# Pooled attention and two feed-forward layers on one core: the opening redone, attention stages reordered, a pass's weights fetched before it

## What is computed

```
attention (B=8, H=8, S=576, D=64):  k_p, v_p = mean of k, v over groups of 8 rows        (72 rows left)
    p = softmax(q k_p^T / sqrt(D));  attended = p v_p        -> x, 4608 tokens x 512
layer 1:  h = x w_in;   y = (h * sigmoid(h)) w_out            (512 -> 2048 -> 512)
layer 2:  h = y w_in2;  out = (h * clip(h + 3, 0, 6) / 6) w_out2
```

## Time and profile before

| | |
|---|---|
| median of 3 runs | 1788.66 us (1784.32 to 1789.85) |
| profiled execution, its own time | 1785.52 us |
| its span, first to last instruction | 1783.4 us |
| busy: PE, DVE, ACT, POOL | 96%, 58%, 41%, 17% |
| mean granted clock of PE | 0.977 |

### The profile page before, as it was taken

The page is one execution under the profiler, slowest core; times in us unless marked ns, Lnnn a source line. Parts: engine busy times, 40 slices in busy tenths (PEclk is TensorE's granted clock), DMA queues, the critical chain, the costliest instruction groups (busy, mean ns, idle before and its releaser), DMA issues. The chain is left out here.

```text
span 1783.4 us, 27222 instructions
## 1 busy us (share of the span) xinstructions
PE 1703.2 (96%) x10992; PEld 1518.4 (85%) x10992; DVE 1041.1 (58%) x1578; ACT 728.3 (41%) x1180; POOL 307.3 (17%) x421
## 2 busy tenths in 40 slices
PE   5778999999999999999999999999999999999999
PEld 4668788788788989999999889999999899999998
DVE  6745565565465456555555765555555776666664
ACT  3544454454454443333333444433444533333332
POOL 3563254254220240000000320000001400000000
PEclk7889999999999999999999999999999999999999
DMA  7232243243221232222222231111112332212221
GB/s 172 75 106 82 82 112 89 81 118 97 81 84 45 95 119 71 72 83 81 86 95 90 75 107 48 48 48 48 48 48 71 92 122 71 71 71 71 77 78 60
DMA packets 130293, 145.95 MB, mean 82 GB/s; under 512 B 47992, under 2 KB 74872, under 8 KB 130168
## 3 DMA queue, kind: packets, MB, share of 16 engines
q1 hardware_dynamic: 80424, 128.08, 22.2%
q10 hardware_dynamic: 49744, 16.13, 3.6%
HBM read 96.99 MB, written 47.19 MB: 81 GB/s over the span
## 5 line engine op out<-in xcount | busy, mean ns | idle before, releaser
L992 DVE TENSOR_TENSOR x_sum<-xy,x_sum 128x256 f32<-128x256 f32 x144 | 60.7, 422 | 227.7 <-ACT x_sum L749 227.7
L1025 DVE TENSOR_TENSOR g_lo<-g_raw,g_hi 128x1024 fp32r<-128x1024 f32 x144 | 184.2, 1281 | 6.4 <-ACT g_raw L761 6.4
L531 PE MATMUL xy<-xr_hi,w1r_hi 128*128 128x256 f32 x576 | 167.8, 291 | 11.7 <-DVE x_sum L992 6.3
L749 ACT COPY x_sum<-xy 128x256 f32<-128x256 f32 x144 | 52.5, 366 | 299.7 <-PE xy L533 299.6
L605 PE MATMUL acc<-g_hi,w_hi 128*128 128x512 f32 x400 | 173.3, 433 | 0.0
L532 PE MATMUL xy<-xr_lo,w1r_hi 128*128 128x256 f32 x576 | 163.6, 284 | 0.0
L533 PE MATMUL xy<-xr_hi,w1r_lo 128*128 128x256 f32 x576 | 163.6, 284 | 0.0
L606 PE MATMUL acc<-g_lo,w_hi 128*128 128x512 f32 x400 | 162.1, 405 | 0.0
L607 PE MATMUL acc<-g_hi,w_lo 128*128 128x512 f32 x400 | 161.3, 403 | 0.0
L1016 DVE TENSOR_TENSOR g_raw<-zw,x_sum 128x512 f32<-128x512 f32 x144 | 99.2, 689 | 102.4 <-PE zw L533 102.4
L461 POOL TENSOR_TENSOR w_sum<-w_raw 128x256 f32<-128x256 f32 x16 | 17.2, 1074 | 771.4 <-DMA w_raw<-in_moe_w_in_dram 771.4
(11 more groups left out here) (184 smaller groups left out, 4851.8 us busy)
## 6 DMA issues: line engine op xcount, KB each, us to landing
partial<-y_stage SPq DMA_DIRECT2D x72, 256.0 KB, 2.0
y_part<-partial SPq DMA_DIRECT2D x18, 1024.0 KB, 5.9
x_raw<-first_layer_t SPq DMA_DIRECT2D x18, 1024.0 KB, 7.7
x_raw<-attended_t SPq DMA_DIRECT2D x10, 1024.0 KB, 8.1
first_layer_t<-y_stage SPq DMA_DIRECT2D x36, 256.0 KB, 2.0
out_dram<-y_stage SPq DMA_DIRECT2D x36, 256.0 KB, 2.0
w_raw<-in_moe_w_in_dram SPq DMA_DIRECT2D x16, 512.0 KB, 4.4
y_stage<-in_moe_w_out_dram SPq DMA_DIRECT2D x32, 256.0 KB, 2.6
```

Source lines behind the costliest of these rows:

```text
L531: nc.tensor.matmul(dst, s_hi[i], m_hi[i], start=first and i == 0, stop=False, skip_group_check=True)
L1025: nc.vector.tensor_tensor(g_lo[:, p], g_raw[:, p % 2], g_hi[:, p].bitcast(fp32), ALU.subtract)\
```

## The change

Five things are done.

1. **The opening.** Queries of tiles 0 and 1 are loaded from ACT's queue. Of the four key pairs DVE reduces three and POOL adds the third (`k_first_added`). Values of batch 0 and keys of batch 1 are both summed on PE, in four groups of eight matmuls with 128 columns each (`sum_v`, `sum_k_next`), placed between the softmax's stages. Other banks of PSUM are used, so that scores need not wait for one another's readers.
2. **The fifth tile** of batch 0: its scores stay in the opening, but its `shift`, `exp`, `norm`, `pt` and `pv` are in step 0. Its result goes straight into `x_raw`, so step 1 loads no x.
3. **The plans.** `kt` moves to place 1 and to bank 0, beside `qt` 0 in bank 1; stages of tiles 0 to 2 move one place forward, `pt` and `pv` of tiles 0 to 3 mostly one place back; `pt` and `pv` of tile 4 stay; `exp` of tile 4 moves from U+9 to U+14.
4. **The next x** is prepared at U+22 instead of U+21 in steps 0 to 6 (behind `pt` of tile 4, which is at U+22 too and comes first in each engine's program) and at U+6 instead of U+10 in the others.
5. **Weights.** In a pass's last step pairs 0 and 1 of the next `w_in` are rounded at places 4 and 5 and split by POOL, pairs 2 and 3 rounded at U+12 and U+16 and split by DVE at U+18 and U+21. The first four pieces of the next `w_out` are then loaded into `w1_raw`, in the same step; the other four follow in the next. For pass 0 two pieces of `w_out` are loaded in the opening, and rounding goes on to place U.

```diff
-PLAN = {2: [("kt",)], 3: [("qt", 0)], 4: [("s", 0)], 5: [("qt", 1)], 6: [("s", 1)], 7: [("qt", 2)], U: [("s", 2)],
+PLAN = {1: [("kt",), ("qt", 0)], 3: [("s", 0)], 4: [("qt", 1)], 5: [("s", 1)], 6: [("qt", 2)], 7: [("s", 2)],
         U + 2: [("qt", 3)], U + 4: [("s", 3), ("exp", 0, 3)], U + 5: [("norm", 0), ("qt", 4)], U + 6: [("exp", 3, 4)],
-        U + 7: [("s", 4)], U + 8: [("norm", 1)], U + 9: [("exp", 4, 5), ("pt", 0)], U + 10: [("norm", 2)],
-        U + 11: [("pv", 0)], U + 12: [("pt", 1), ("norm", 3)], U + 14: [("pv", 1)], U + 15: [("pt", 2), ("norm", 4)],
-        U + 17: [("pv", 2)], U + 18: [("pt", 3)], U + 20: [("pv", 3)], U + 22: [("pt", 4)], U + 24: [("pv", 4)]}
-PLAN_FIRST = {**PLAN, 1: [("kt",), ("norm", -1)], 2: [("qt", 0)], 3: [("s", 0)], 4: [("pt", -1)], 5: [("pv", -1), ("qt", 1)]}
+        U + 7: [("s", 4)], U + 8: [("norm", 1)], U + 10: [("norm", 2), ("pt", 0)], U + 12: [("pv", 0), ("norm", 3)],
+        U + 13: [("pt", 1)], U + 14: [("exp", 4, 5)], U + 15: [("pv", 1)], U + 16: [("pt", 2), ("norm", 4)],
+        U + 18: [("pv", 2)], U + 19: [("pt", 3)], U + 21: [("pv", 3)], U + 22: [("pt", 4)], U + 24: [("pv", 4)]}
+PLAN_FIRST = {1: [("kt",), ("qt", 0)], 2: [("exp", -1, 0)], 3: [("norm", -1), ("s", 0)], 4: [("pt", -1), ("qt", 1)],
+              5: [("pv", -1), ("s", 1)], 6: [("qt", 2)], 7: [("s", 2)], U + 2: [("qt", 3)], U + 4: [("s", 3), ("exp", 0, 3)],
+              U + 5: [("norm", 0), ("qt", 4)], U + 6: [("exp", 3, 4)], U + 7: [("s", 4)], U + 8: [("norm", 1)],
+              U + 10: [("norm", 2)], U + 12: [("pt", 0), ("norm", 3)], U + 14: [("pv", 0), ("exp", 4, 5)],
+              U + 15: [("pt", 1)], U + 16: [("norm", 4)], U + 17: [("pv", 1), ("pt", 2)], U + 19: [("pv", 2), ("pt", 3)],
+              U + 21: [("pv", 3)], U + 22: [("pt", 4)], U + 24: [("pv", 4)]}
-W1_AT = [U + 1, U + 3, U + 21, U + 24]
+W1_ROUND_AT = [4, 5, U + 12, U + 16]
+W1_SPLIT_AT = [U + 18, U + 21]
+W2_FIRST_AT = [3, 4, 5, 6, 7, U]
 def next_at(s):
-    return U + 21 if s < FREE else U + 10
+    return U + 22 if s < FREE else U + 6
...
+        def w2_source(ps, f):
+            if ps == 0:
+                return y_stage[:, f % 2], w2_loaded[f % 2]
+            c = f % 4
+            return w1_raw[:, c // 2, c % 2 * 2:c % 2 * 2 + 2, :].rearrange("p a n -> p (a n)"), w2_loaded[c]
...
+            def load_w2(ps, f):
+                dst, landed = w2_source(ps, f)
+                if ps == 0:
                     if f >= 2:
-                        sp.wait_ge(w2_split, ps * NF + f - 1)
-                    elif ps:
-                        sp.wait_ge(y_stored[f], 16 * 2 * NB * ps)
+                        sp.wait_ge(w2_split, f - 1)
+                elif f < 4:
+                    sp.wait_ge(w1_split, w1_splits(ps, 2 + f // 2))
+                else:
+                    sp.wait_ge(w2_split, ps * NF + f - 3)
...
                 if ps and blk == 0:
-                    load_w2(ps)
+                    for f in range(4, NF):
+                        load_w2(ps, f)
...
                     load_w1(ps + 1, 3)
+                    for f in range(4):
+                        load_w2(ps + 1, f)
...
-            for n, width in enumerate((4 * D, 2 * D, D)):          # POOL, values of batch 0
-                dst = v_first[:, :, :width] if width > D else v_pool[:]
-                nc.gpsimd.tensor_tensor(dst, v_first[:, :, :width], v_first[:, :, width:2 * width], ALU.add)
+            for p in range(NPAIR):
+                sums(0, p)
+            for f in range(NF):
+                if f >= NF - 2:
+                    pool_head(f - (NF - 2))
+                split_w2(0, f)
+            for n in range(2, HEADS):
+                pool_head(n)
+            for ps in range(1, PASSES):
+                sums(ps, 0)
+                sums(ps, 1)
+                split_w1(ps, 0)
+                split_w1(ps, 1)
+                sums(ps, 2)
+                sums(ps, 3)
...
+                first_queries(0)                                   # PE, the opening
+                first_queries(1)
+                transpose_k(acc[1])
+                first_queries(2)
+                first_scores(0)
+                first_scores(1)
+                first_queries(3)
+                first_scores(2)
+                sum_v(0)
+                first_scores(3)
+                sum_v(1)
+                first_turn(0)
+                sum_v(2)
+                sum_v(3)
+                first_turn(1)
+                first_values(0)
+                sum_k_next(0)
+                first_turn(2)
+                first_values(1)
+                sum_k_next(1)
+                sum_k_next(2)
+                first_turn(3)
+                first_values(2)
+                first_queries(FIRST)
+                sum_k_next(3)
+                first_values(3)
+                first_scores(FIRST)
...
+                for part in range(4):                              # ACT, the end of the opening
+                    round_x(0, part)
+                    if part == 1:
+                        round_w1(0, 1)
...
                 split_w1(0, 0)                                     # DVE, the end of the opening
-                shift(4, first_banks[4], read)
-                sum_x(0)
-                split_w1(0, 2)
+                sum_x_first(0)
+                split_w1(0, 1)
+                sum_x_rest(0)
...
+                    if s == 0 and place == 0:                      # DVE, step 0
+                        shift(FIRST, first_s_banks[FIRST], (first_s_read, first_s_read))
+                        split_w1(0, 2)
```

More of the change, by code:

```diff
@@ L421, in _ @@
                     .then_inc(x_first_stored, 16)
-            load_w2(0)
+            for f in range(2, NF):
+                load_w2(0, f)
+            for n in range(2, H):
+                load_kv(n)
             for s in range(STEPS):
@@ L430, in _ @@
                 if s < FREE:
-                    for n in range(max(2, 2 * H * s), min(2 * H * s + H, HEADS)):
+                    for n in range(max(H, 2 * H * s), min(2 * H * s + H, HEADS)):
                         load_kv(n)
@@ L690, in attend, with sum_k_next @@
                         pe.wait_ge(kv_pooled, 2 * H * (b - 1) + H)
-                    values(pt, t, banks[mine[0]])
+                    values(pt, t, acc[0] if t == FIRST else banks[mine[0]])
+            def sum_k_next(j):
+                pe.wait_ge(k_next_loaded[j], 16)
+                for i in range(POOL):
+                    last = nc.tensor.matmul(ab[0][:SP, j * P:(j + 1) * P], ident[:SP, :SP],
+                                            k_first[:, 2 * j:2 * j + 2, i * D:(i + 1) * D],
+                                            start=i == 0, stop=i == POOL - 1)
+                if j == NK - 1:
+                    last.then_inc(k_next_summed, 1)
@@ new lines, in sum_v, with first_queries @@
+            def sum_v(j):
+                pe.wait_ge(v_loaded[j], 16)
+                for i in range(POOL):
+                    last = nc.tensor.matmul(acc[1][:SP, j * P:(j + 1) * P], ident[:SP, :SP],
+                                            v_first[:, 2 * j:2 * j + 2, i * D:(i + 1) * D],
+                                            start=i == 0, stop=i == POOL - 1)
+                if j == NK - 1:
+                    last.then_inc(v_summed, 1)
+            def first_queries(c):
+                pe.wait_ge(first_q_loaded[c], 16)
+                transpose_q(q_first[:, c], c, first_q_bank[c])
@@ new lines, in first_scores, with first_turn, first_values @@
+            def first_scores(c):
+                pe.wait_ge(first_qt_copied, c + 1)
+                scores(qt_first[:, c], c, first_s_banks[c])
+            def first_turn(c):
+                if c < 2:
+                    pe.wait_ge(first_s_read, 2 * (c + 2))
+                pe.wait_ge(p_ready, c + 1)
+                transpose_p(c, first_p_banks[c])
+            def first_values(c):
+                pe.wait_ge(first_pt_copied, 2 * c + 2)
+                if c == 2:
+                    pe.wait_ge(first_x_copied, 1)
+                elif c == 3:
+                    pe.wait_ge(first_x_copied, 2)
+                values(pt_first[:, c % 2], c, first_v_bank[c])
@@ L718, in attend_first @@
-                pe.wait_ge(k_next_loaded, 16)
-                for i in range(POOL):
-                    last = nc.tensor.matmul(acc[1][:SP], ident[:SP, :SP], k_first[:, :, i * D:(i + 1) * D],
-                                            start=i == 0, stop=i == POOL - 1)
-                last.then_inc(k_next_summed, 1)
+                first_scores(0)
[3 more added lines that the diff above has]
+                sum_v(0)
+                pe.wait_ge(first_s_read, 2)
@@ L886, in attend_first @@
             def attend_first():
+                for c in range(2):
+                    act.dma_start(q_first[:, c], q_rows(c)).then_inc(first_q_loaded[c], 16)
                 act.wait_ge(ident_ready, 2)
@@ L918, in copy_x @@
```

(20 more changed lines are left out.)

259 lines of the change are left out of this document (135 added, 124 removed).

## The result

The changed kernel takes 1724.1 us (median of four runs, 1721.64 to 1724.13), the kernel before 1786.74 (1784.32 to 1789.85): ratio 0.9645, 95% interval 0.9631 to 0.9658. It is 62.6 us faster. The forecast was 1713, so 11 us too low, inside its range.

The account below looks back on a forecast made before the run. PE, busy 96% of the span, was taken as the bound, with time won only at its waits or half clock. 36 + 11 + 9 + 18 = 74 us off 1785.5 gave 1711.5, put down as 1713; range 1700 to 1726.

Parts of the forecast that it names:

- Steps 1 to 6: Tile 4's pv wait, qt waits and the clock's falls go: 6.0 us a step, 36 us; bounds 22 and 38.
- The rival of the staying fall: In steps 1 to 6 the clock still falls without the waits: 14 us less, 1727 us; chance 0.12.
- Opening: Up to step 0's first chunk: step 0 starts at 50 us for 58.8, 9 us won; bounds 13 won, 5 lost.
- Step 0: First step, with the fifth tile's rest: 72 us for 90.2, 18 us won; bounds 9 and 26.
- Values: Step 0, pv of tile 0 waiting for POOL's pooled value heads: 0 to 2 us.
- Clock: Step 0, half clock behind the wait for the fifth tile's pt: about 3 us.
- The fifth tile: Step 0: PE waits 4 us for its pt behind DVE's work, and 1 us more at its pv.
- The bare 62.4: Step 0's earlier 90.2 us without its 20.7 us of waits and its 7 us of half clock.
- Starts of passes: Passes 1 to 3: 8.9 us of waits and two clock falls go, 11 us won; bounds 5 and 12.3.
- The front gives little: Opening as before, and step 0 with new waits gains only 9 us: 1731 us; chance 0.17.
- That tile 4 is held by the store: Tile 4 still waits 2.9 us, ACT held by tile 2's store: 33 us less, 1746 us; chance 0.06.
- x comes too late: The next x, begun later behind pt, is late in each of seven steps: slower, say 1800 us; chance 0.03.

Follow-up runs that it names:

- before_x22: Kernel before, with only the next x in steps 0 to 6 rounded by ACT at U+22 instead of U+21; 1750.39 us.
- after_x21_two: Changed kernel, with two of the four roundings of the next x at U+21, the other two at U+22, in steps 0 to 6; 1731.59 us.
- after_x21: Changed kernel, with the next x in steps 0 to 6 rounded at U+21 again, ahead of tile 4's pt; 1765.22 us.
- after_k_last: Changed kernel, with all four sums of batch 1's keys on PE moved behind the opening's last scores; 1720.17 us.
- after_starts: Changed kernel, with w_out pieces 2 and 3 loaded behind the step's stores, and ACT's pass 2 roundings of pairs 0 and 1 at places 5 and 7; 1724.52 us.
- after_pool_less: Changed kernel, with POOL subtracting only part of the low halves' columns from pass 1 on, so part of the computation is left out; 1716.28 us.
- own_dve_k: after_v_own plus the moves of after_shift and after_k_last, and pair 3's split behind the fifth tile's norm in step 0; 1713.75 us.
- own_dve_k3: own_dve_k, with one of the four key sums left in the opening ahead of tile 3's turn; 1711.15 us.
- after_v_own: Changed kernel, with pooled key and value buffers swapped from batch 1's values on, and POOL's value heads and SP's loads reordered; 1716.67 us.
- after_shift: Changed kernel, with DVE's shift of the fifth tile's scores at the end of the opening instead of behind chain 0 of step 0; 1723.43 us.
- after_v_pool: Changed kernel, with batch 0's values pooled by POOL's wide additions again instead of by PE's sums; 1732.30 us.

## Why the prediction came out as it did

**Steps 1 to 6: right, with its reason.** Forecast 60.6 us a step, measured 60.7. Both halves of the term were tried apart: before_x22 takes away the wait alone and wins wait and clock together; after_x21_two puts back 0.76 us of wait and no clock; after_x21 puts back both. The rival of the staying fall (0.12) is wrong for these steps. The Trainium skill's rule on short idles (TensorE: Matmul & The Clock Gate, "A second HAM failure mode") is not borne out in them: waits of up to 0.48 us in steps 1 to 6 of before_x22 and of 0.76 in those of after_x21_two left the clock at 1.00. The prediction's own premise, that waits of 0.4 to 1.7 us have no fall behind them, is not safe either: among the open ends below are waits of 1.44 and 1.76 us with one. The term didn't need it, since no wait above 0.5 us was left in these steps. Its lower bound has a slip: without the clock it comes to 6 x 3.5 = 21 us, not 22.

**Opening: right in size, partly by luck.** Forecast 50.0 us, measured 50.5. First scores came at 15.07 us, not at 12.3: of the 3.4 us that were to be won there 0.6 came, near the bound of 0 that I had named. By the length of its matmuls (0.42 us for 128 columns up to 19.7 us, 0.27 behind it) PE was at full clock from 19.8 us on, about where 7 us of half clock after 12.3 would have ended: luck, since only 4.8 us at half clock followed the first scores. The last `pv` ended at 44.4 for 43.6; the x chain took 5.0 us, as read from the earlier trace rows. after_k_last shows that the stretch is bound by PE's work, with DVE close by: with 7.2 us of sums moved away the last `pv` ends 5.3 us sooner, and PE then waits for DVE, 1.6 us in two waits.

**Step 0: the term that was mis-sized.** It was "62.4 + 6 + 4 = 72", and it measured 81.0. The mechanisms were all there, the sizes weren't:
- Values: forecast 0 to 2 us, measured 5.67; "two heads are done ahead, six are left behind the last piece (at U + 1.5 us)". The six heads of 2.1 us are right. The last piece ends at 94.4 us, 8.8 us behind U and not 1.5. POOL's last wait for ACT's rounding is over at 85.51 us, at U; behind it come three splits and the two heads that I had taken as done ahead, which stand in POOL's program between pieces six, seven and eight.
- Clock: forecast 3 to 4 us; three stretches at half clock, in which PE was busy for 3.37, 5.80 and 4.87 us, lose half of these 14.0, 7.0 us. I had counted a fall behind one wait, the fifth tile's. The wait for pooled values brought a second, and the 5.13 us in which PE waits for x at the end of the opening a third.
- The fifth tile: forecast 4 + 1 us, measured 2.77 and nothing at its `pv`; a `qt` wait of 1.6 us wasn't in the sum.

The bare 62.4, waits of 12.1 (by PE's timeline, seven in all) and 7.0 of clock make 81.5. That the two largest are causes is shown by taking them away: step 0 takes 75.3 us without the values' wait, and 72.0 with the fifth tile's put right as well.

**Starts of passes: mechanism half right.** Both falls of the clock went (3.4 us), and 8.9 us of waits became 4.8, where I had left 1 us "for ACT, which is crowded". It is hardly ACT: it is DVE's `split_g`, held by POOL's subtractions. The largest wait, 1.77 us, lies in the last step of pass 2, beside the split that the change gave to POOL. after_starts leaves ACT and the stores only 0.4 us of the 4.8, after_pool_less shows POOL.

**The other rivals.** "The front gives little" (0.17, 1731) is half right: the opening gave its 8.3 us, but step 0 had the new waits that this rival named, and gave 9 us less than forecast. That tile 4 is held by the store (0.06) and that x comes too late (0.03) didn't happen: no wait for `x_sum` or `xs_lo` stands at the starts of steps 1 to 6.

**The sum.** 1711.5 and 3 us make 1714.5, not the 1713 that was put down. The four terms were 74 us and came to 61.1; the miss has no part that made up for another.

**What stays open.** Why a wait of 1.44 us brings a fall in own_dve_k while one of 1.34 us at the same place in after_k_last brings none, nor one of 2.43 us in step 0 of own_dve_k3. There are more such pairs at one place. The `qt` wait of step 0 has a fall behind it at 1.81 us (after_x21), 1.89 (own_dve_k) and 1.91 (after_v_own), and none at 1.80 (after_starts), 1.82 (after_shift) and 2.16 (after_v_pool). The wait in the last step of pass 2 has one at 1.76 us (after_starts) and none at 1.77 (changed kernel). The length of a wait doesn't decide alone; no run here tells what else does. So a term for the clock behind a wait of 1.4 to 2.4 us is a chance, not a price, and part of the difference between two kernels' executions can be such falls alone.

## What to carry to other kernels

When the engine that bounds a kernel waits once per step at the same place, look at the order of the queue of whoever it waits for before redesigning stages: one number was worth 36 of 63 us here. Count a long wait (2.9 us and more in these steps) at its length and the half clock behind it, and fill the gap with work that has to be done anyway. When an edit gains nothing, look whether a later wait has grown, as in after_shift. Work "done ahead" in a queue is ahead only if nothing before it in that queue waits. And work moved to POOL wasn't free for DVE here: `split_g`, with both inputs in SBUF, waited out POOL's subtractions that it fell on.

## What the runs showed of the hardware

- Without a wait above 0.5 us in steps 1 to 6 the granted clock stays at 1.00 (2.4 GHz) for 441 us on end (the changed kernel); with a 3.6 us wait in each step it is at half (1.2 GHz) for 3.4 and 6.8 us in turns (after_x21).
- Between the two the same wait can have a fall behind it or not: 1.81 us with, 1.82 us without, at one place (after_x21, after_shift).
- Idle time of PE in the opening costs more than its length: 6.4 us of waiting from 21.6 us on was followed by 17 us of half clock (after_v_pool), and with the stretch filled with sums there was none before 50.5 us (the changed kernel).
- A DVE operation of 0.2 us took 3.20 beside POOL's wide additions (after_v_pool), and `split_g` 1.8 to 3.2 for 1.2 us beside POOL's work (the changed kernel). An operation of DVE with one input in PSUM isn't slowed: all 144 of the form at 1314.24 us take 0.42 to 0.43 us.
